# Two early units ahead of each mixture's tables, and two experts' weights loaded in the convolution stage

## The reference

```python
x_unf = x_pad[:, idx, :].reshape(B, S, K, H, group)
x = np.einsum('hk,bskhg->bshg', softmax(weight), x_unf).reshape(B * S, D)

def moe(x, w_gate, w1, w2, ...):            # first: rows with x @ w_skip > 0 only
    logits = x @ w_gate                     # second: + modality_bias[modality_id]
    e_idx = np.argmax(logits, axis=1)
    gate_w = softmax(logits)[arange, e_idx]
    for e in range(E):
        mask = e_idx == e
        h = np.maximum(x[mask] @ w1[e], 0.0)
        y[mask] = gate_w[mask, None] * (h @ w2[e])
    # first: out[do_compute] = xc + y, second: out = y
```

## Time and profile before

| | us |
|---|---|
| median of 3 runs | 1223.38 (1221.72 to 1226.15) |
| profiled execution, its own time | 1223.26 |
| its span, first to last instruction | 1221.6 |
| PE busy | 1121.5 |
| POOL, DVE, ACT busy | 462.2, 661.2, 457.6 |
| mean granted PE clock | 0.942 |

### The profile page before, as it was taken

How to read it: one execution, slowest core, us unless ns; L and a number is a source line. 1 busy time by engine, 2 the same in 40 slices (tenths; PEclk the granted TensorE clock), 3 DMA queues, 4 the chain that set the end, 5 groups by cost and what they waited for, 6 DMA issues and landing times.

```text
span 1221.6 us, 27087 instructions
## 1 busy us (share of the span) xinstructions
PE 1121.5 (92%) x8431; PEld 1081.7 (89%) x8432; DVE 661.2 (54%) x1942; ACT 457.6 (37%) x867; POOL 462.2 (38%) x582
## 2 busy tenths in 40 slices
PE   5888989719999999999959999999999999999996
PEld 5777777609999999999949999999999999999996
DVE  4545555556867777777855444444444444444444
ACT  2423333214545535544515333333333333333333
POOL 5345555553433244424424322222333322333224
PEclk9878878858999999999989999999999999999998
DMA  5644444135333243243225111111111111111110
GB/s 153 177 122 124 127 126 121 51 109 141 112 100 102 65 116 111 60 120 114 59 89 161 40 40 42 45 40 40 40 40 43 40 43 40 40 40 40 41 45 22
DMA packets 85357, 97.13 MB, mean 80 GB/s; under 512 B 26706, under 2 KB 76198, under 8 KB 85330
## 3 DMA queue, kind: packets, MB, share of 16 engines
q1 hardware_dynamic: 68138, 66.26, 20.3%
q0 software_dynamic: 15072, 28.47, 7.3%
q10 hardware_dynamic: 2120, 2.09, 0.5%
HBM read 65.01 MB, written 33.54 MB: 81 GB/s over the span
## 4 chain that ended last, share of the span: by engine, by line
PE 82%; issue 8%; DVE 3%; another core or an unknown queue 3%; ACT 1%; SPq 1%; DMA 1%; POOL 0%; ACTq 0%; DVEq 0%; POOLq 0%
PE banks L1033 36%; PE banks L1046 22%; PE banks L1042 10%; PE banks L503 2%; DVE valid L1161 1%; PE banks L501 1%; PE banks L1025 1%; PE banks L1022 1%; PE banks L1023 1%; PE banks L218 1%; PE banks L515 1%; PE banks L516 1%; PE banks L528 1%; PE banks L219 1%
## 5 line engine op out<-in xcount | busy, mean ns | idle before, releaser
L1033 PE MATMUL banks<-xt,w_up 128*128 128x256 f32 x3600 | 450.6, 284 | 2.6 <-ACT xt L1106 2.3
L1033 PEld LDWEIGHTS banks<-xt,w_up 128*128 128x128 f32 x3600 | 447.2, 190 | 3.7 <-ACT xt L1106 2.6
L1046 PE MATMUL banks<-w_dn,hid_hi 128*128 128x384 f32 (+1 forms) x1440 | 434.7, 365 | 0.0
L1125 ACT ACTIVATE hid_hi<-banks 128x512 fp32r<-128x512 f32 x360 | 213.9, 597 | 502.8 <-PE banks L1033 468.3
L1042 PE MATMUL banks<-w_dn,hid_lo 128*128 128x192 f32 (+1 forms) x1440 | 356.4, 255 | 0.0
L1219 DVE SCALAR_TENSOR_TENSOR hid_lo<-banks,hid_hi 128x512 fp32r<-128x512 f32 x360 | 245.1, 690 | 193.8 <-ACT hid_hi L1125 160.5
L1042 PEld LDWEIGHTS banks<-w_dn,hid_lo 128*128 128x128 f32 x1440 | 273.8, 191 | 0.0
L1046 PEld LDWEIGHTS banks<-w_dn,hid_hi 128*128 128x128 f32 x1440 | 270.4, 188 | 0.0
L328 POOL DMA_INDIRECT out<-y_both,idx x114 | 112.1, 983 | 247.6 <-DVE y_both L1212 217.2
L975 POOL TENSOR_TENSOR split<-ahead,split 128x256 fp32r<-128x256 f32 x94 | 65.3, 695 | 285.7 <-ACT split L1110 285.5
L480 POOL DMA_INDIRECT buckets<-rows,idx x128 | 121.3, 947 | 120.0 <-DVE idx L799 70.7
(11 more groups left out here) (198 smaller groups left out, 1208.7 us busy)
## 6 DMA issues: line engine op xcount, KB each, us to landing
ahead<-buckets SPq DMA_DIRECT2D x94, 202.0 KB
x_in<-in_x SPq DMA_DIRECT2D x16, 672.0 KB
stage<-in_w SPq DMA_DIRECT2D x11, 768.0 KB
kept<-buckets SPq DMA_DIRECT2D x33, 202.0 KB
stage<-in_w SPq DMA_DIRECT2D x11, 512.0 KB
stage<-in_w SPq DMA_DIRECT2D x22, 256.0 KB
w_turned<-in_w_t SPq DMA_DIRECT2D x8, 512.0 KB
w_turned<-in_w_t SPq DMA_DIRECT2D x8, 256.0 KB
```

The costliest lines, as they stand in the source:

```text
L1033: mm = nc.tensor.matmul(o, w_up[:, slot, w, f * P:(f + 1) * P], xt[:, a * UNIT:(a + 1) * UNIT], start=(m == 0), stop=(m == len(terms) - 1))
L1046: mm = nc.tensor.matmul(p_y[:, t, 0:2 * COLS], hid_hi[:, f, c], w_dn[:, slot, f, :, 0:COLS], start=(f == 0), stop=(f == FT - 1))
L1125: nc.scalar.activation(hid_hi[:, 2 * b:2 * b + 2, :], p_h[:, b % HB, :].rearrange("p (f c) -> p f c", f=2), ACT.Relu).then_inc(hi_done, 1)
```

## The change

The first two units of each mixture ("early") take rows of the mixture's expert 0 that are known before its tables are, and PE, ACT, DVE and POOL have them written out ahead of the wait for `tables_done`. `know_early` looks whether 512 rows are there: for mixture 1 before the destinations of group 14, for mixture 2 at the stage's end. If not, two units of spare empty rows are taken. It moves `base`, so that the tables count the rest, and `seg_start` is shifted by 2. `has` is set for the first two experts instead of one, since both experts' weights are loaded before the tables: expert 0's near the start of the convolution stage, expert 1's behind x of group 3, and in mixture 2 expert 1's behind the first early rows. `tables` becomes `table_counts` and `table_units`, which stand on DVE between the parts of the early units. All eight tails are written by SP, behind the second early unit's rows. The routing of mixture 1's last unit (`End`) moves into mixture 2's early units. PE gets six filling matmuls before the last ranks, and four instead of ten before mixture 1.

```diff
+    EARLY = 2
+    SPARE = CL * CAP
@@ table_counts (was tables)
-            link(nc.vector.memset(has[:, 0:1], 1.0))
+            link(nc.vector.memset(has[:, 0:2], 1.0))
@@ table_units
+                link(nc.vector.tensor_reduce(tabf[:, 10, :], seg_t[:, 1, :, :], AX.X, ALU.add))
+            nc.vector.tensor_scalar(seg_start[layer][:, :], tabf[:, 10, :], float(EARLY), None, ALU.add)
@@ write_tails
-            for e in experts:
+            for e in range(E):
@@ conv_stage, sync
+                load_weights(sp, 0)
                 load_turned(sp, 0, 0)
                 load(2, 0, 2)
                 load(3, 0, 3)
-                load_weights(sp, 0)
+                sp.wait_ge(consts, N_CONSTS)
+                for u in range(EARLY):
+                    sp.dma_start(buckets[SPARE + u * UNIT:SPARE + (u + 1) * UNIT, :]..., empty[:, :, :]...)
+                sp.wait_ge(w_hi, HI_PIECES)
+                sp.wait_ge(w_lo, LO_PIECES)
+                sp.wait_ge(w_lo2, LO2_PIECES)
+                load_weights(sp, 1)
                 with sp.Fori(1, B) as b:
                     for k in range(GB):
                         load(b * GB + k, b, k)
-                write_tails(sp, 0, range(0, E, 2), tails_sp[0])
@@ conv_stage, gpsimd
+                for q in range(HI_PIECES):
+                    pool.wait_ge(w_hi, q + 1)
+                    split_lo(pool, nc.gpsimd, 0, q, w_lo if q < N_UP else w_lo2)
                 def scatter(i, b, k):
+                    if isinstance(i, int) and i == 1:
+                        pool.wait_ge(fold_lo_done, 2)
+                        put_fold(pool, 0, 0)
@@ conv_stage, vector
+                def know_early(layer):
+                    at = layer * E
+                    low = base[0:1, at:at + 1]
+                    taken, row = early_f[:, layer, 0:1], early_f[:, layer, 1:2]
+                    link(nc.vector.tensor_tensor(taken, carry[0:1, at:at + 1], low, ALU.subtract))
+                    link(nc.vector.tensor_scalar(taken, taken, float(EARLY * UNIT), float(EARLY * UNIT), ALU.is_ge, ALU.mult))
+                    link(nc.vector.tensor_scalar(row, taken, ..., float(SPARE), ALU.mult, ALU.add))
+                    nc.vector.tensor_copy(early_row[layer][:, 0:1], row)
+                    link(nc.vector.tensor_tensor(low, low, taken, ALU.add))
+                    nc.vector.tensor_copy(early_row[layer][:, 1:2], low).then_inc(early_known[layer], 1)
                 read_logits(NG - 1, B - 1, GB - 1, 0)
+                know_early(0)
                 dest(NG - 2, B - 1, GB - 2)
...
                 dest(NG - 1, B - 1, GB - 1)
-                tables(dve, 0)
-                ...split_lo of all eight pieces
+                know_early(1)
+                know_tails(dve, 0)
                 fold_lo(dve, p_fold, NG - 1, E - 1, 1)
@@ mixture, sync
+                sp.wait_ge(early_known[layer], 1)
+                at = sp.value_load(early_row[layer][0:1, 0:1], ...)
+                follows = sp.value_load(early_row[layer][0:1, 1:2], ...)
+                if last:
+                    sp.wait_ge(split_done_of[0], units_before + 2)
+                else:
+                    sp.wait_ge(spare_written, 16 * EARLY)
+                    for k in range(GB):
+                        sp.wait_ge(scattered[k], 16 * TG * (B if k < 2 else B - 1))
+                sp.dma_start(ahead[:, :, :], rows_at(at, 0)).then_inc(ahead_loaded, 16)
+                if last:
+                    load_weights(sp, E + 1)
+                    sp.wait_ge(y_read_of[0], units_before + 1)
+                keep(rows_at(at, 0))
+                sp.wait_ge(split_done, 1)
+                sp.dma_start(ahead[:, :, :], rows_at(at, UNIT)).then_inc(ahead_loaded, 16)
+                write_tails(sp, layer)
+                ...wait for the last sends or scatters
+                sp.wait_ge(split_done, 2)
+                sp.dma_start(ahead[:, :, :], rows_at(follows, 0)).then_inc(ahead_loaded, 16)
+                sp.wait_ge(y_read, 2)
+                keep(rows_at(at, UNIT))
                 sp.wait_ge(tables_done[layer], 1)
@@ mixture, gpsimd
-                split_rows(0)
+                if last:
+                    split_rows(0)
+                    split_rows(1)
+                    end.send(pool)
+                for g in range(EARLY):
+                    if not last:
+                        send(g)
+                    split_rows(g + 2)
+                    if last:
+                        pool.wait_ge(y_read, g + 2)
+                        store_rows(pool, idx1, y_out, out, sent_done)
                 pool.wait_ge(tables_done[layer], 1)
@@ mixture, tensor
+                transpose(0)
+                begin(segs_before if last else 0)
+                for g in range(EARLY):
+                    early_unit(g, 0)      # as unit, but transpose(g + 1) in the middle of down,
+                                          # and end.ranks in the middle of up(0) of mixture 2
                 pe.wait_ge(tables_done[layer], 1)
@@ mixture, vector
+                if last:
+                    end.route(dve)
+                    hidden(0, 0)
+                    hidden(0, 1)
+                    end.dest(dve)
+                    nc.vector.memset(valid[:, :], 0.0).then_inc(y_read, 1)
+                    know_tails(dve, 1)
+                    hidden(0, 2)
+                    hidden(0, 3)
+                    table_counts(dve, 1)
+                    ...
+                    finish(0)
+                    for b in range(NB):
+                        hidden(1, b)
+                    table_units(dve, 1)
+                    finish(1)
+                else:
+                    nc.vector.memset(valid[:, :], 0.0).then_inc(y_read, 1)
+                    split_rows(0)
+                    hidden(0, 0)
+                    split_rows(1)
+                    for b in range(1, NB):
+                        hidden(0, b)
+                    route(0)
+                    table_counts(dve, 0)
+                    dest(0)
+                    finish(0)
+                    for b in range(NB):
+                        hidden(1, b)
+                    route(1)
+                    table_units(dve, 0)
+                    dest(1)
+                    finish(1)
                 dve.wait_ge(tables_done[layer], 1)
```

More of the change, by code:

```diff
@@ L599, in tensor @@
                 fold_turn(pe, p_fold, NG - 1)
+                for _ in range(FILL_RANK):
+                    nc.tensor.matmul(p_conv[:, 0, :], ones[:, :], ones_wide, start=True, stop=True)
                 ranks(NG - 1, B - 1, GB - 1)
@@ L966, in sync @@
                                 unit(g)
-                if not last:
-                    write_tails(sp, 1, range(0, E, 2), tails_sp[1])
             def gpsimd(pool):
@@ L1126, in unit @@
                                              ACT.Relu).then_inc(hi_done, 1)
+                def unit(g, n, k, slot, first):
+                    hidden(g)
                     read_xt(g + 1)
```

332 lines of the change are left out of this document (196 added, 136 removed).

## The result

The changed kernel takes 1266.06 us (median, 1262.68 to 1268.41), the kernel before 1222.55 beside it (1219.82 to 1226.15): the ratio is 1.0352, 95% interval 1.0315 to 1.0389. It is slower by 43.5 us, 12 more than the 31 forecast. The profiled execution has a span of 1266.7, 45.1 more than the 1221.6 of before.

The account below looks back on a forecast made before the run. PE's units were taken to set the time. The terms 0.5 - 5 + 10.5 - 9.8 + 35.1 sum to +31.3, on 1223.3 giving 1254.6, stated as 1254; own range 1248 to 1260, wider range 1238 to 1264.

Parts of the forecast that it names:

- The sign: Whole kernel: the change makes it slower, chance 0.94.
- the places: Where the change was to be read: the two PE holes, any added unit, any segment made short.
- the convolution stage: Convolution stage: moved weight splits fit POOL's slack, `know_early` delays the last scatters 0.9; +0.5, bounds -2 and +3.
- The one-unit segment: Mixture 1, expert 0's segment cut to one unit: PE waits for the next expert's weights; +10.5, bounds 8 and 13.
- Some 2 late, of which I take 1 as felt: Mixture 1, weight load following the short segment: arrives some 2 after ACT wants it, 1 counted.
- The first hole: PE's hole before mixture 1: early units start in it, slowed by slow issue; -5, bounds -15 and 0.
- PE isn't held: Rival, hole before mixture 1: PE runs unhindered there, -15 for -5, total 1244; chance 0.22.
- The second hole: Hole between the mixtures: early units start sooner, 2.2 lost to missing rows; -9.8, bounds -13.5 and -6.
- The end: Mixture 2's end: two added units and three one-unit segments wait for weights; +35.1, bounds +20 and +38.
- Weights hidden: Rival, mixture 2's short segments: only the two added units cost, 19.9 for 35.1, total 1239; chance 0.08.
- the faster case: Rival: mixture 2 keeps 57 units, nothing is added at its end, total 1219.5; chance 0.04.
- slow stretch takes more: Rival: tails or moved writes hold unit 2's rows, or POOL's splits delay the convolution stage; +8, 1262, chance 0.12.

Follow-up runs that it names:

- late_57: Changed kernel with POOL's eight pieces moved behind group 2's scatters, second weight load behind loads of x, and 57 units in mixture 2; ratio 1.0086.
- splits_on_dve_2: Changed kernel with POOL's eight pieces made by DVE behind the convolution stage and the second weight load behind the tails, at the lower clock; 1260.2 us.
- second pair: Second traces of the kernel before and the changed kernel, both unchanged; 1224.71 us (one run) and ratio 1.0338.
- end_57: Changed kernel with only expert 0 forced into mixture 2's segments and the second segment's weights loaded after the tables; ratio 0.9967.
- before_again: Kernel before, unchanged, traced again beside the follow-up runs; 1224.71 us (one run).
- before_pool_copy: Kernel before with ten added one-input copies on POOL ahead of the first scatters; ratio 0.9998.
- before_has2: Kernel before with the first two experts put into `has` in mixture 2, nothing else; ratio 1.0279.
- mixture2_only: Changed kernel with mixture 1 as before, early units in mixture 2 only, one expert forced there, second segment's weights loaded after the tables; ratio 0.9968.
- spare_rows: Changed kernel with mixture 1's early units working on empty rows, so expert 0 keeps three units; 1275.24 us against 1265.34 for the changed kernel.
- spread_splits_2: Changed kernel with POOL's pieces singly between scatters of groups 0 to 3, second weight load behind loads of x, at the lower clock; 1251.2 us.

## Why the prediction was wrong

**The sign, the places and the counts were right**; the measured 1266 is 12 above the forecast 1254 and 2 above the upper end of the range. What the input does to the tables (33 and 59 units, segments of 54, 1, 1, 1, twelve sets of weights) was read off exactly.

**The step that failed: the convolution stage, +0.5 with a bound of +3, measured +5.4.** It asked whether POOL's pieces fit beside POOL's scatters ("the stage has slack for it on POOL") and never what a POOL piece does to DVE. The traces show DVE's operation on the path held for 2.82, four later ones for 0.2 to 0.7 longer each, first destinations 4.6 later, and the difference kept from burst to burst: 37.6 for 33.0 at the first, 93.7 for 88.5 at the fourth, 252.9 for 246.6 at the last. Of the 14 that the sum missed by, this term makes 4.9, and it is the only one outside its own bounds in both pairs. The timeline of POOL and DVE in the changed kernel:

```profile
25.06 4.95 POOL L209 TENSOR_TENSOR w_up<-stage,w_up 128x512 fp32r<-128x512 f32 x4
...
27.03 0.23 DVE L796 TENSOR_TENSOR logit<-logit,banks 112x68 f32<-112x68 f32 x1
27.29 2.81 DVE L802 TENSOR_TENSOR logit<-logit,rows 112x64 f32<-112x64 f32 x1
...
32.12 3.91 POOL L209 TENSOR_TENSOR w_dn<-stage,w_dn 128x384 fp32r<-128x384 f32 x4 [2.11 <-ACT w_dn L205]
...
32.23 1.03 DVE L813 TENSOR_TENSOR pick<-hot,takes 112x128 bf16<-112x128 f32 x1
33.49 0.66 DVE L820 TENSOR_SCALAR den<-den 112x16 f32<-112x16 f32 x1
...
34.47 0.64 DVE L822 TENSOR_TENSOR inv<-inv,takes 112x16 f32<-112x16 f32 x1
```

The prediction did weigh the rule for this, at the end of the kernel, where both engines' pieces overlap; it never took it to the place where pieces were new. The Trainium skill (SBUF — State Buffer, Who interferes with whom) says that a DVE instruction with two on-chip inputs contends with a GpSimd one that reads on-chip memory, for ports that it calls an exclusive lock, and that a DVE instruction with at most one such input outside its two-port modes does not. L796 and L802 are this pair: 0.23 and 2.81. `den` (L820) has one such input and is held all the same, so by that rule it would have to run in a two-port mode, which no trace shows.

How long a hold lasts differs. L802 waits past two ends of pieces, until the last of the four is done; so do the holds of 2.04, 4.42 and 7.40. The four behind it end each about as one piece of 0.98 ends (33.26, 34.15, 35.11, 36.18), though these pieces follow without a gap too. What decides between the two, no run shows.

The five holds add 4.5, and the first burst is 4.6 late. That they happen, move with the pieces (`late_57`) and go with them (`splits_on_dve_2`) is shown up to the fourth burst; that nothing else is in the 5.4 at the last one is not.

**The one-unit segment, +10.5 in 8 to 13, measured 15.1, and 12.2 in the second pair.** The mechanism was right: PE waits for the last POOL piece (9.04, forecast 9.5). Two things were mis-sized. The sum has nothing for the clock behind PE's waits: the 40 matmuls of unit 2, behind 7.15 without work, take 6.83, and those of unit 3, behind the 9.04, take 6.49, both for 4.96 (granted clock 0.71 for 303.2 to 310.2 and 0.75 for 324.4 to 331.0), 3.4 in all. And the load behind the wait comes late: unit 5's rows are asked for only behind it (329.68), land at 334.5, and ACT's pieces follow at 334.93, 10.5 after the unit's start where it was 7.7. "Some 2 late, of which I take 1 as felt" became 2.8 late. From unit 3's start to unit 6's, 4.0 were lost in the first pair and 1.1 in the second, 1.5 of them by the clock; what is left for the late load is no more than the pairs differ by.

**The first hole, -5, measured -2.4.** PE started up(0) at 261.16, not held at first: 32 of 40 matmuls had started by 265.8, when a stretch of slow issue began, and the last eight took until 276. SP's eight tails lay across it, 17.87 long. With the stage's 5.4 the tables were due at 299.5 and were ready at 300.2. The rest is 2.97 in the chain ("issue") between them and unit 2, where I took 1 for PE's loads of registers. The rival "PE isn't held" is out at this clock; at the higher one, in `end_57`, PE is not held, and unit 2 comes 15.8 earlier, the size of the rival's -15.

```profile
261.16 4.95 PE L1117 MATMUL banks<-xt,w_up 128*128 128x256 f32 x32
...
262.85 17.87 SPq L361 DMA_DIRECT2D buckets<-empty  x8
...
269.98 0.37 PE L1117 MATMUL banks<-xt,w_up 128*128 128x256 f32 x1 [1.82 <-issue]
...
300.04 0.18 DVE L348 CAST unit_row<-unit_s 1x69 int32<-1x69 f32 x1
...
303.20 1.00 PE L1117 MATMUL banks<-xt,w_up 128*128 128x256 f32 x3 [7.15 <-issue]
```

**The second hole, -9.8, measured -7.5, and -9.3 in the second pair.** Moved by the 18.5 that mixture 1 is late, up(0) was due at 647.6 and came at 647.55; unit 2 was due at 673.4 and came at 675.29. The stall is the forecast one: eight tails, then rows.

```profile
655.29 8.07 SPq L361 DMA_DIRECT2D buckets<-empty  x8
...
665.38 0.36 SPq L1015 DMA_DIRECT2D ahead<-buckets  x1
...
667.84 0.52 ACT L1217 ACTIVATE split<-ahead 128x384 fp32r<-128x384 f32 x1 [2.56 <-DMA ahead<-buckets]
```

POOL has the rows split at 670.0 (forecast 669.5 with the shift), and the tables are ready at 670.4 (671.5). But the turns of unit 2's rows stand in the middle of down(1), and its second half, behind them, runs at half the clock, 1.2 GHz, and ends at 675.3: I had it end at 672.5. The windows (columns as in the earlier trace rows) show PE nearly idle and then the clock at 0.50:

```profile
666.00:670.00 4.00, 0.94 (x7) 0.70 (x6) 3.73 (x16) 0.52 (x1) 1.43 (x2) 0.88 0.22 52
670.00:673.00 3.00, 2.88 (x14) 2.91 (x15) 0.54 (x3) 0.81 (x1) 1.97 (x2) 0.50 0.11 39
```

**The end, +35.1, measured 34.2 and 36.5**, and +33.9 from its one line alone. Distances 14.07 and 18.77 for 13.8 and 17.6. "Weights hidden" is out, and so is the faster case. The rival "slow stretch takes more" (+8, 1262) came nearest; it named "the splits on POOL delay the conv stage" beside other things and gave it 12 in 100.

## What to carry to other kernels

When work moves to another engine, price it twice: what it takes there, and what it does to the engines beside it, at the step that has no slack. Here one DVE operation of 0.22 took 2.81 beside POOL's pieces. Compare such a version at the steps right behind the moved work, not at the end of a long stage, where other things had moved the last scatter by more. And measure at each clock that the kernel meets: the early units of mixture 1 gained 15.8 up to unit 2 at one and lost 2.95 at the other. Work out with the real inputs what a table does with a forced entry: one more flag in `has` cost 34 us. Before a stall is put down to a queue of transfers, look at what the in-order engine between them is waiting for.

## What the runs showed of the hardware

- **The clock in the convolution stage differed between times on the same chip.** For 40 to 240 us (40 to 200 in the second) the windows of `before_again` and `before_pool_copy` show (busy us of each engine and its instructions, granted clock, DMA share, GB/s):

```profile
40.00:240.00 200.00, 174.92 (x1076) 151.64 (x1075) 108.58 (x388) 65.30 (x141) 98.51 (x105) 0.80 0.42 115
```

```profile
40.00:200.00 160.00, 142.06 (x1087) 121.64 (x1086) 112.85 (x401) 65.30 (x142) 100.68 (x107) 0.95 0.53 145
```

  The same number of matmuls in 200 us at a mean of 0.80, in 160 at 0.95. The bursts of eight behind the first become runs of 16 and 30 scatters, and the kernel is some 46 us shorter. What decides it, no run shows.
- **Stretches of slow issue stand behind bursts of scatters**: all engines but POOL go on only every 0.7 us or so, for 1 to 4 us behind each burst of eight at the lower clock, and for 9.7 (265.84 to 275.55) in the changed kernel's last burst of 16. At the higher clock most bursts have none. Whether the rows written or the issuing of the scatters makes them is open; a kernel with the last bursts left out was not run.
- **TensorE's first groups run slower for longer in some traces of either kernel.** The first matmul of the convolution starts at 15.2 to 15.6 in all of them. But in `before_has2`, `mixture2_only`, `spare_rows` and `spread_splits_2` the same matmuls still take 0.88 at 21 us where others have been at 0.52 since 17 us or before: TensorE goes to its higher clock later there. The page's granted clock does not show it; for the first 20 us it is 1.00 in either case.

```profile
21.02 0.88 PE L501 MATMUL banks<-x_in,band 118*112 118x168 f32 x2
```

```profile
19.05 0.52 PE L501 MATMUL banks<-x_in,band 118*112 118x168 f32 x2
```

  (`before_has2`, then the kernel before.) The first burst is then some 3.5 late, with no edit near: 36.3 in place of 32.8 for `before_has2`, 41.0 for 37.7 for `spare_rows`. It is as large as the effect that was looked for, so a first burst is to be compared by what DVE's operations take, not by its time alone.
